# Issuing the gathers of an expert loop one tile later in GpSimd's order

## The reference

```python
logits = x @ w_gate + modality_bias[modality_id]
e_idx = np.argmax(logits, axis=1)
gate_w = softmax(logits)[np.arange(N), e_idx]
for e in range(E):
    mask = e_idx == e
    h = np.maximum(x[mask] @ w1[e], 0.0)        # 512 -> 1024
    out[mask] = gate_w[mask, None] * (h @ w2[e])  # 1024 -> 512
```

## Time and profile before

| | us |
|---|---|
| median of three executions | 932.46 |
| the profiled execution | 932.91 |
| its span, first to last instruction | 931.1 |

### The profile page before, as it was taken

One profiled execution on the slowest core, in us unless ns is written; L12 is line 12 of the kernel. 1 busy time (PEld: TensorE's weight loads), 2 busy tenths in 40 slices (PEclk: granted clock), 3 DMA queues, 4 the chain that ended last, 5 costly groups with the idle time before them and its releaser, 6 DMA issues.

```text
span 931.1 us, 16050 instructions
## 1 busy us (share of the span) xinstructions
PE 860.2 (92%) x4845; PEld 733.0 (79%) x4846; DVE 506.2 (54%) x1023; ACT 429.5 (46%) x1186; POOL 232.5 (25%) x218
## 2 busy tenths in 40 slices
PE   5888888879999999999999999997699999999995
PEld 3666667758998998988998998986578888888883
DVE  6899999944665555555555555576762111111110
ACT  3777777764555445445345345454043222222221
POOL 1567776543211001001001002053311111111110
PEclk9799999978999999999999999999799999999998
DMA  5555555221000000000000000220061111111100
GB/s 108 148 148 143 150 147 149 72 56 45 26 22 35 1 1 34 0 0 34 0 0 34 0 0 34 91 91 0 34 219 42 45 45 37 40 45 45 45 34 13
DMA packets 88197, 51.57 MB, mean 55 GB/s; under 512 B 64480, under 2 KB 77280, under 8 KB 88160
## 3 DMA queue, kind: packets, MB, share of 16 engines
q1 hardware_dynamic: 85040, 41.16, 15.8%
q0 software_dynamic: 3120, 9.96, 3.2%
HBM read 41.67 MB, written 9.70 MB: 55 GB/s over the span
## 4 chain that ended last, share of the span: by engine, by line
PE 72%; DVE 16%; issue 5%; ACT 2%; DMA 2%; POOL 1%; DVEq 1%; SPq 0%; ACTq 0%; POOLq 0%
PE ps L1440 8%; PE ps L1442 8%; PE ps L1441 8%; PE ps L1330 7%; PE ps L1331 7%; PE ps L1332 7%; PE ps L1306 6%; PE ps L1305 6%; PE ps L1311 6%; DVE ssum L903 3%; DVE smax L893 3%; DVE kdz L878 2%; DMA vwin<-in_v_dram 2%; PE ps L1463 2%; PE ps L1347 1%
## 5 line engine op out<-in xcount | busy, mean ns | idle before, releaser
L992 DVE TENSOR_SCALAR Tb<-Eb 128x384 f32<-128x384 f32 x96 | 41.4, 431 | 133.9 <-ACT Eb L737 133.9
L737 ACT ACTIVATE Eb<-ps 128x384 f32<-128x384 f32 x96 | 47.1, 491 | 141.5 <-PE ps L1311 141.3
L667 ACT ACTIVATE prob<-ps,nmax 96x111 f32<-96x111 f32 (+1 forms) x256 | 87.7, 355 | 23.7 <-DVE nmax L897 23.4
L1306 PE MATMUL ps<-xh,WA 128*128 128x384 f32 x288 | 98.2, 341 | 0.0
L1305 PE MATMUL ps<-xh,WA 128*128 128x384 f32 x288 | 97.7, 339 | 0.0
L562 POOL TENSOR_TENSOR xl<-xT,xh 128x384 fp32r<-128x384 f32 x24 | 26.8, 1144 | 280.4 <-ACT xh L709 280.4
L1330 PE MATMUL ps<-WA,gh 128*128 128x512 f32 x216 | 87.1, 403 | 2.4 <-DVE gl L951 2.4
L1332 PE MATMUL ps<-WA,gl 128*128 128x512 f32 x216 | 85.4, 395 | 0.0
L1331 PE MATMUL ps<-WA,gh 128*128 128x512 f32 x216 | 85.2, 394 | 0.0
L746 ACT ACTIVATE Rb<-Tb 128x384 f32<-128x384 f32 x96 | 50.5, 526 | 73.5 <-DVE Tb L994 73.5
L1171 DVE TENSOR_TENSOR hTl<-ps,hTh 128x1024 fp32r<-128x1024 f32 x19 | 23.2, 1223 | 97.5 <-ACT hTh L800 97.5
(11 more groups left out here) (218 smaller groups left out, 2030.8 us busy)
## 6 DMA issues: line engine op xcount, KB each, us to landing
wsraw<-in_moe_w_dram SPq DMA_DIRECT2D x32, 256.0 KB, 3.3
vwin<-in_v_dram SPq DMA_DIRECT2D x32, 166.5 KB
qraw<-in_q_dram SPq DMA_DIRECT2D x32, 144.0 KB, 3.0
kraw<-in_k_dram SPq DMA_DIRECT2D x32, 144.0 KB, 3.0
vdraw<-in_v_dram SPq DMA_DIRECT2D x32, 144.0 KB
y_rows<-yrow SPq DMA_DIRECT2D x6, 768.0 KB, 3.6
wraw<-in_moe_w_in_dram SPq DMA_DIRECT2D x12, 256.0 KB, 5.6
wraw<-in_moe_w_out_dram SPq DMA_DIRECT2D x12, 256.0 KB, 3.4
```

What stands on the lines that cost most here:

```text
L667: last = act.activation(prob[0:np_, a.s6, n * w:(n + 1) * w], ps[0:np_, o:o + w], ACT.Exp, scale=sc, bias=nmax[0:np_, a.s6, n:n + 1], accu ...
L1306: pe.matmul(dst, lo, xh[:, kk, :], start=False, stop=False)
```

## The change

GpSimd issues two gathers ahead instead of three, and then alternates `gather(t + 2)`, `scatter(t)`. Tiles, tables, waits and all other engines' streams stay as they are.

```diff
-            AHEAD = 3
-            for t in range(AHEAD):
-                gather(t)
+            gather(0)
+            gather(1)
             pool.wait_ge(rt_tables, 1)
             n_tiles = pool.value_load(tab_n[0:1, 0:1], min_val=NTOK, max_val=NSLOT)
-
-            def gather_if_used(t):
-
-                if t <= NTOK:
-                    gather(t)
-                elif t <= NSLOT:
-                    with pool.If(n_tiles > t - 1):
-                        gather(t)
-
             for t in range(NTOK):
-                gather_if_used(t + AHEAD)
+                if t + 2 <= NTOK:
+                    gather(t + 2)
+                elif t + 2 <= NSLOT:
+                    with pool.If(n_tiles > t + 1):
+                        gather(t + 2)
                 scatter(t)
             pool.wait_ge(scat, 16 * NTOK)
             for t in range(NTOK, NSLOT):
-                gather_if_used(t + AHEAD)
+                if t + 2 <= NSLOT:
+                    with pool.If(n_tiles > t + 1):
+                        gather(t + 2)
                 with pool.If(n_tiles > t):
                     scatter(t)
                     pool.wait_ge(scat, 16 * t + 16)
```

## The result

| | us |
|---|---|
| before, median of 4 | 932.37 |
| after, median of 4 (946.5 to 948.1) | 946.88 |
| predicted (range) | 935.7 (933.0 to 941.5) |

The ratio after to before is 1.0156, with a 95% interval of 1.014 to 1.0173. The direction was forecast, the size was not: 14.5 us instead of 3.2, and outside the range. Three further executions of the changed kernel took 945.0 to 947.3 us.

What follows compares the result with a forecast made beforehand. TensorE's own instructions were taken as the bound; 1.01 + g + 3.3 + 0.10 against 4.49 us of slack, with g = 0.24, gave 1.5 + 0.56 + 0.66 + 0.34 + 0.15 = 3.2 us, so 935.7 us, range 933.0 to 941.5.

Steps and rivals of the forecast that it cites:

- The bound: Expert loop, 703 to 912 us: TensorE is busy 209.00 of 209.00 us and never waits for a gather.
- the order of GpSimd's stream: On GpSimd, gathers 3 to 19 each move past one scatter; before, no scatter was held up by a gather.
- the 4.49 us to the transposes: Steady tiles: time from scatter t's start to tile t+3's transposes on TensorE, taken as the gather's deadline.
- The gap g = 0.24 us: On GpSimd, between the scatter's end and the next gather's start; unknown in the trace, taken as 0.24 us.
- a full turnaround: Rival: GpSimd starts a DMA only once the one before is through, g 0.4 to 0.83; 942 us, chance 0.20.
- The landing behind a scatter, 3.3 us: Tiles 4 to 17: the gather lands 3.2 to 3.5 us after its start, median 3.3, taken over for the changed order.
- Tiles 18 and 19 dearer: The last two gathers land after 3.7 and 3.8 us, so they pause TensorE 0.56 and 0.66 us.
- A late scatter, 0.34 us: One scatter, at 839.36, left only 4.15 us to the transposes; if that recurs once, 0.34 us more.
- The branch, 0.15 us: Behind the last scatter GpSimd steps over one unused branch more, 0.15 us at the very end.
- The tail's clock: Rival: TensorE's clock drop after 912 us may shift, up to 1.7 us either way; gain, by this or something unseen, 0.03.
- TensorE wakes up ... Together 0.10: TensorE after a late landing: 0.04 us until the transposes start, which take 0.66 instead of 0.60; 0.10 us together.
- what would show it: Expected signs: TensorE waits for `xg` in most tiles, about 3 us in sum; time lost elsewhere would show the forecast wrong.

Runs made afterwards that it cites:

- experiment 5: Kernel before, with gather t+3 also waiting on GpSimd for tile t's result but still ahead of scatter t: 932.62 us, ratio 0.9999.
- 8: Kernel before, gather t+3 delayed by waiting for tile t's result and three fills, TensorE's register read moved to the loop body's head: 936.64 us, ratio 1.005.

## Why the prediction was wrong

- *The bound, the order of GpSimd's stream and the 4.49 us to the transposes*: right as read. The loop was bound by TensorE, and the gather did become the last to arrive. That these 4.49 us are the deadline was wrong, see below.
- *The gap g = 0.24 us*: nearly right, 0.30. By the prediction's own working that is 0.06 x 16 = 1 us more. The rival "a full turnaround", with g from 0.4 on, comes nearest in its total (942, up to 946) but for the wrong reason: g was below its 0.4.
- *The landing behind a scatter, 3.3 us*: right. *Tiles 18 and 19 dearer*: right. *A late scatter, 0.34 us*: none came. *The branch, 0.15 us*: fits. *The tail's clock*: nothing seen; from the last scatter but one to the last it is 10.64 us, against 10.66 before.
- *"TensorE wakes up ... Together 0.10"*: this term of the sum failed. It counted the way from the landing to the transposes (0.04) and their longer run (0.06). It should have gone on to the first matmul behind them, with the register read that the queue still has to do: from landing to product 853.43 - 0.04 = 853.39 to 854.43, 1.04 us. Without a late landing the product starts 0.35 us behind the transposes' start. I took that start as the deadline, put the queue's work behind the wait at nothing without a word, and it costs 0.6 us per tile. The right sum, on the same clock: 1.01 + 0.30 + 3.3 + 1.04 = 5.65 against 4.49 + 0.35 = 4.84, that is 0.81 per tile and 13.8 us in 17, plus the last tiles.
- The view that would have shown it was at hand: the queue's own rows beside the engine's. The list of TensorE's busy instructions leaves register instructions out. The question that wasn't asked is what TensorE's queue does between the instruction that now waits and the next one that computes.

In "what would show it" the prediction named waits of about 3 us in sum. The pauses in front of the transposes, 4.3 us in 17 tiles, are just that, with the 1 us for the larger gap. The other 10.5 us stand behind them. So the direction was no luck, but the part of the loss that was foreseen is less than a third of it. The section also named, as a sign of being wrong, time lost elsewhere than in these waits; that sign came.

## What to carry to other kernels

When a wait becomes real, add to it what the same engine's queue has to do between that wait and the next computing instruction. Here that was the reading of a register; address arithmetic, branches and further waits belong to the same question but were not tested. As long as the queue is far enough ahead of the engine this is free, and no busy view shows it. Once the operand comes too late for that, the read lies open in every iteration, here with 0.6 us. A slack is therefore to be counted back from the next computing instruction that depends on that queue, and register reads belong ahead of the wait that may be late. Where two DMAs on one queue compete, the one with a deadline goes first: with the gather ahead of the scatter even the later release cost nothing (experiment 5).

## What the runs showed of the hardware

- GpSimd starts an indirect DMA 0.30 or 0.31 us behind the end of another, in all 17 pairs.
- A gather directly behind a scatter lands about as soon as one alone: tiles 3 to 19 took 3.2 to 3.9 us in the changed kernel, tiles 4 to 19 took 3.2 to 3.8 before. The last tiles land latest, in experiments 5 and 8 after 4.3 us; why was not looked into.
- Where it lies open, a register read costs TensorE 0.62 to 0.65 us, with the register instructions that go with it; its load itself takes 0.30 to 0.31 us in the changed kernel. Hidden behind the matmuls in the kernel before, the load mostly took 0.54 us (0.30 to 0.57), which cost nothing. TensorE's queue had a lead of about 3 us over the array in the kernel before, and one such read more per tile fitted into it without cost (933.08 against 932.96 us).
